# Attention, routed experts and a feed-forward layer in one Trainium2 kernel: values loaded in thirds on one queue, routing in groups of three, single scatters between key copies, and a new order of the last tile

## What is computed

```python
k_sum = k.reshape(B, H, nb, block, D).max(axis=3)
v_sum = v.reshape(B, H, nb, block, D).mean(axis=3)
...
a = a / (np.sum(a, axis=-1, keepdims=True) + 1e-09)
out = np.matmul(a, v_all)
...
logits = x @ w_gate
noise_scale = np.log1p(np.exp(x @ w_noise))
noisy_logits = logits + noise_scale * noise
top2 = np.argpartition(-noisy_logits, 2, axis=1)[:, :2]
...
h = np.maximum(x[mask] @ w1[e], 0.0)
out[mask] += top2_w[mask, k, None] * (h @ w2[e])
...
g = s * (r * r) + b
return g @ w_out
```

## Time and profile before

| | us |
|---|---|
| median of 3 runs (703.12 to 707.35) | 706.74 |
| the profiled execution, its own time | 703.65 |
| its span on the core | 702.0 |
| PE busy in the span | 683.7 (97%) |
| PE's first product of the first expert starts | 103.31 |

### The profile page before, as it was taken

The page is one execution under the profiler, slowest core; times in us unless marked ns, Lnnn a source line. Parts: engine busy times, 40 slices in busy tenths (PEclk is TensorE's granted clock), DMA queues, the critical chain, the costliest instruction groups (busy, mean ns, idle before and its releaser), DMA issues.

```text
span 702.0 us, 10455 instructions
## 1 busy us (share of the span) xinstructions
PE 683.7 (97%) x4065; PEld 569.8 (81%) x4065; DVE 261.0 (37%) x551; ACT 216.1 (31%) x499; POOL 309.4 (44%) x278
## 2 busy tenths in 40 slices
PE   8898989999999999999999999999999999999998
PEld 3466789788888888888999899888888888888886
DVE  6467766431230212312121244944505235051330
ACT  2458955221220311203131313411324113141231
POOL 1415745567988396697889562302021020200000
PEclk9999968999999999999999999999999999999999
DMA  9996433699979195792979599932012020100001
GB/s 261 255 289 183 168 136 134 221 397 362 405 258 400 54 388 197 254 382 76 384 249 397 183 336 315 379 113 61 1 60 61 1 60 1 45 15 1 0 1 60
DMA packets 55966, 132.34 MB, mean 189 GB/s; under 512 B 8712, under 2 KB 11016, under 8 KB 55920
## 3 DMA queue, kind: packets, MB, share of 16 engines
q0 software_dynamic: 28144, 82.77, 33.7%
q1 hardware_dynamic: 27155, 47.77, 20.9%
q10 hardware_dynamic: 621, 1.18, 0.7%
HBM read 104.79 MB, written 25.97 MB: 186 GB/s over the span
## 4 chain that ended last, share of the span: by engine, by line
PE 91%; issue 2%; DMA 2%; ACT 2%; DVE 1%; POOL 1%; SPq 0%; POOLq 0%
PE ps L380 27%; PE ps L382 27%; PE ps L381 27%; PE ps L1531 2%; PE ps L1464 1%; PE ps L1419 1%; DMA v_all<-v_all 1%; PE ps L1447 1%; PE ps L1391 1%; ACT prob L693 1%; PE ps L1427 1%; PE ps L1669 1%; PE ps L1456 1%; POOL kwin L567 1%; POOL x_sorted L582 1%
## 5 line engine op out<-in xcount | busy, mean ns | idle before, releaser
L546 POOL TENSOR_TENSOR w_lo<-w_raw,w_hi 128x1024 fp32r<-128x1024 f32 x56 | 134.2, 2416 | 20.5 <-DMA w_hi<-in_w_pieces_dram 19.7
L967 DVE SCALAR_TENSOR_TENSOR h_lo<-ps,h_hi 128x448 fp32r<-128x448 f32 (+2 forms) x64 | 36.7, 574 | 197.2 <-ACT h_hi L704 197.2
L380 PE MATMUL ps<-x_hi,w_hi 128*128 128x448 f32 (+2 forms) x256 | 88.2, 345 | 0.0
L704 ACT ACTIVATE h_hi<-ps 128x448 fp32r<-128x448 f32 (+2 forms) x64 | 32.3, 505 | 181.0 <-PE ps L382 181.0
L381 PE MATMUL ps<-x_lo,w_hi 128*128 128x448 f32 (+2 forms) x256 | 88.0, 344 | 0.0
L382 PE MATMUL ps<-x_hi,w_lo 128*128 128x448 f32 (+2 forms) x256 | 88.0, 344 | 0.0
L380 PE MATMUL ps<-w_hi,h_hi 128*128 128x512 f32 x216 | 86.8, 402 | 0.0
L382 PE MATMUL ps<-w_hi,h_lo 128*128 128x512 f32 x216 | 84.5, 391 | 0.0
L381 PE MATMUL ps<-w_lo,h_hi 128*128 128x512 f32 x216 | 84.5, 391 | 0.0
L1313 DVE SCALAR_TENSOR_TENSOR sqr<-relu,sbb 128x512 f32<-128x512 f32 x48 | 36.2, 754 | 112.9 <-ACT relu L838 112.2
L381 PE MATMUL ps<-y_lo,w_hi 128*128 128x512 f32 (+1 forms) x200 | 76.1, 381 | 0.0
(11 more groups left out here) (228 smaller groups left out, 1125.0 us busy)
## 6 DMA issues: line engine op xcount, KB each, us to landing
w_raw<-in_w_pieces_dram POOLq DMA_DIRECT2D x56, 512.0 KB, 13.8
w_hi<-in_w_pieces_dram POOLq DMA_DIRECT2D x56, 512.0 KB, 15.3
xb<-x_sorted SPq DMA_DIRECT2D x25, 256.0 KB, 7.5
y_sorted<-ysb SPq DMA_DIRECT2D x25, 256.0 KB, 2.0
x_sorted<-zrow SPq DMA_DIRECT2D x7, 896.0 KB, 15.0
w_raw<-in_w_pieces_dram SPq DMA_DIRECT2D x8, 512.0 KB, 4.7
w_hi<-in_w_in_dram POOLq DMA_DIRECT2D x8, 512.0 KB, 7.8
w_raw<-in_w_in_dram SPq DMA_DIRECT2D x8, 512.0 KB, 8.3
```

Of the source, the lines that this page charges most:

```text
L380: pe.matmul(acc, l_hi, r_hi, start=start, stop=False, skip_group_check=True)
L546: pool.tensor_tensor(piece(w_lo, slot, k), piece(w_raw, slot, k), piece(w_hi, slot, k).bitcast(F32), ALU.subtract).then_inc(pieces_split, 1)
L704: act.activation(hi[:, i // FT % 2, i % FT, 0:rows], ps[:, i % FT, 0:rows], ACT.Relu).then_inc(sg.hhi_ready, 1)
L967: dve.scalar_tensor_tensor(out=lo[:, at, i % FT, 0:rows], in0=ps[:, i % FT, 0:rows], scalar=0.0, in1=hi[:, at, i % FT, 0:rows].bitcast(F32 ...
```

## The change

The mask is loaded ahead of the keys. ACT issues no transfers any more: all values of the first batch are loaded by SP, in three pieces of 4, 4 and 4 windows (the last made of three transfers), each with a semaphore of its own. The rest of the queries waits on SP until the second piece has landed, and the keys of the second batch now come before its values. PE takes each third of the means as it lands. POOL copies four rows of means itself, in two copies, and one of the spreading DMAs is gone. PE's order for tiles 0 to 2 is new, the 50 warming products become 39. Routing goes in four groups of three tiles, `EARLY_TILES` is 6. The first 12 scatters are issued one by one between POOL's key copies, each behind a wait on PE's progress. In the last tile PE turns the probabilities, then x of tile 10, then does the values, ranks and logits; DVE normalises before it reads. Behind it ACT's last logarithm stands ahead of its first `up_early`, DVE's second `up_early` ahead of `split_first(2)`, and the last ranks stand inside `down_early(0)`.

The core of the diff:

```diff
@@ -73,11 +73,10 @@
 HPT = HPB // KD
-GROUP_OF = ((0, 4), (4, 7), (7, 10), (10, 12))
-RANK_BANK = (7, 7, 2, 7)
+GROUP_OF = ((0, 3), (3, 6), (6, 9), (9, 12))
 RAW_AT = (6, 6, 6, 6, 7, 8)
-ROUND_AT = (8, 9, 11)
-GMAX = 4
+ROUND_AT = (8, 10, 11)
+GMAX = 3
@@ -385,16 +384,19 @@
             sp.dma_start(cst[:, :], consts[:, P:]).then_inc(c_in, 16)
+            sp.dma_start(msk[0:80, :], masks[0:80, 0:4 * P]).then_inc(m_in, 16)
             load_keys(sp, 0)
-            sp.dma_start(msk[0:80, :], masks[0:80, 0:4 * P]).then_inc(m_in, 16)
...
             sp.dma_start(ident[:, :], consts[:, 0:P]).then_inc(id_in, 16)
-            load_windows(sp, 0, 0, HPB // 2, v_in[0])
+            for i in range(HPT):
+                load_windows(sp, 0, i * KD, min((i + 1) * KD, HPB - 1), v_third[i])
+            load_last_window(sp, 0, v_third[HPT - 1])
+            sp.dma_start(wg[:, :, :], w_gate.rearrange("(k p) e -> p k e", p=P)).then_inc(g_in, 16)
+            sp.wait_ge(v_third[HPT - 2], 16)
             load_queries(sp, 0, 1)
-            sp.dma_start(wg[:, :, :], w_gate.rearrange("(k p) e -> p k e", p=P)).then_inc(g_in, 16)
-            load_windows(sp, 1, 0, HPB - 1, v_in[1])
-            load_last_window(sp, 1, v_in[1])
             load_keys(sp, 1)
+            load_windows(sp, 1, 0, HPB - 1, v_in)
+            load_last_window(sp, 1, v_in)
@@ -568,19 +570,22 @@
             def spread_means(b):
-                pool.wait_ge(rows_ready, b + 1)
+                pool.wait_ge(rows_ready, 1 if b == 0 else 3)
...
                     pool.wait_ge(pool_win_ready, 4)
-                    pool.tensor_copy(v_all[0][SUMS:COLS, 2:4, :], v_all[0][SUMS:COLS, 0:2, :]).then_inc(rows_copied, 1)
-                for part, (fro, to) in enumerate(((MEANS_BY_DVE[b], 6), (6, HPB))):
+                    for at in (2, 4):
+                        pool.tensor_copy(v_all[0][SUMS:COLS, at:at + 2, :],
+                                         v_all[0][SUMS:COLS, 0, :].unsqueeze(1).broadcast_to([NSUM, 2, DM])).then_inc(rows_copied, 1)
+                for part, (fro, to) in enumerate(((1, 6), (6, HPB))):
+                    if b == 0 and part == 0:
+                        continue
...
-            def scatter(t):
-                for c in range(2):
-                    pool.indirect_dma_start(out=x_sorted, out_offset=bass.IndirectOffsetOnAxis(pos_i[:, t, c:c + 1], 0),
-                                            in_=x_sb[:, t, :], in_offset=None).then_inc(scattered, 16)
+            def scatter(t, c):
+                pool.indirect_dma_start(out=x_sorted, out_offset=bass.IndirectOffsetOnAxis(pos_i[:, t, c:c + 1], 0),
+                                        in_=x_sb[:, t, :], in_offset=None).then_inc(scattered, 16)
@@ -590,21 +595,41 @@
             key_windows(8)
-            key_windows(9)
-            key_windows(10)
...
             pool.wait_ge(pos_ready, 1)
-            for t in range(*GROUP_OF[0]):
-                if t == 2:
-                    key_windows(11)
-                scatter(t)
-            for g in range(1, len(GROUP_OF)):
+            scatter(0, 0)
+            pool.wait_ge(pv_done, 7)
+            scatter(0, 1)
+            key_windows(9)
+            pool.wait_ge(turned, 16)
+            scatter(1, 0)
+            pool.wait_ge(pv_done, 8)
+            scatter(1, 1)
+            key_windows(10)
+            pool.wait_ge(turned, 18)
+            scatter(2, 0)
+            pool.wait_ge(pv_done, 9)
+            scatter(2, 1)
+            pool.wait_ge(pos_ready, 2)
+            scatter(3, 0)
+            key_windows(11)
+            scatter(3, 1)
+            pool.wait_ge(pv_done, 10)
+            scatter(4, 0)
+            pool.wait_ge(scores_done, 12)
+            scatter(4, 1)
+            pool.wait_ge(turned, 22)
+            scatter(5, 0)
+            pool.wait_ge(pv_done, 11)
+            scatter(5, 1)
+            for g in range(2, len(GROUP_OF)):
...
                 for t in range(*GROUP_OF[g]):
-                    scatter(t)
+                    for c in range(2):
+                        scatter(t, c)
@@ -730,9 +755,6 @@
             act.activation(gate[:, :], zrow[:, 0:NT], ACT.Copy)
-            act.wait_ge(k_in[0][PAIRS - 2], 16)
-            load_windows(act, 0, HPB // 2, HPB - 1, v_rest_in)
-            load_last_window(act, 0, v_rest_in)
@@ -740,11 +762,14 @@
                     exps(2)
-                if s >= 1:
+                    act.wait_ge(pv_done, 1)
+                if s >= 3:
...
                                ACT.Copy).then_inc(probT_odd, 1)
+                if s in (1, 2):
+                    x_to_logits(s)
@@ -770,8 +795,8 @@
                 noise_exp(last)
+                noise_ln(last)
                 up_early(0)
-                noise_ln(last)
@@ -1061,50 +1086,50 @@
             mean_weights()
+            masks_to_bf16()
...
             key_sums(1)
-            masks_to_bf16()
...
                     maxima(1)
-                elif s == 1:
-                    maxima(3)
...
                 dve.tensor_copy(probT[0:COLS, 0:4, :], ps[0:COLS, 4, :].rearrange("p (h n) -> p h n", n=P)).then_inc(probT_even, 1)
+                if s == 1:
+                    maxima(3)
                 if s == 0:
+                    copy_means(0)
                     maxima(2)
-                    copy_means(0)
-                    mean_rows(0, 0, 2)
+                    mean_rows(0, 0)
+                    mean_rows(0, 1)
...
                 if s == 4:
-                    mean_rows(1, 0, 1)
+                    mean_rows(1, 0)
                 if s == NT - 1:
-                    route_top(2)
-                    route_chosen(2)
+                    normalise(s)
...
                     read_logits(s - 1)
+                if s in (3, 6, 9):
+                    route_a(s // 3 - 1)
                 if s in (4, 7, 10):
-                    route_a(s // 3 - 1)
-                if s in (5, 8):
                     route_top(s // 3 - 1)
-                if s == 6:
-                    route_c(0)
-                if s == 9:
-                    route_c(1)
+                if s in (5, 8, 11):
+                    route_c(s // 3 - 1)
+                if s == 8:
                     early_count()
-                normalise(s)
-                if s in (5, 8):
+                if s < NT - 1:
+                    normalise(s)
+                if s in (4, 7, 10):
@@ -1117,13 +1142,12 @@
                 x_split(head, i, xa_lo, xa_hi, i, P, 4 + i)
-            route_c(2)
...
             up_early(0)
+            up_early(1)
             split_first(2)
-            up_early(1)
@@ -1475,50 +1500,62 @@
                 for t in range(at, to):
-                    acc = ps[:, RANK_BANK[g], L_RANK + (t - at) * E:L_RANK + (t - at + 1) * E]
+                    acc = ps[:, 7, L_RANK + (t - at) * E:L_RANK + (t - at + 1) * E]
...
-            warm_up(34, 7)
+            warm_up(26, 7)
...
             scores(1)
-            warm_up(8, 7)
+            warm_up(4, 7)
+            mean_third(0, 0)
+            warm_up(6, 7)
...
             scores(2)
-            warm_up(4, 7)
-            means(0)
-            warm_up(4, 7)
+            mean_third(0, 1)
+            mean_third(0, 2)
+            warm_up(3, 7)
             gather_means(0)
+            turn_probs(1)
+            values(0)
             scores(3)
-            values(0)
-            for s in range(1, NT):
-                if 3 < s + 1 < NT:
-                    scores(s + 1)
-                if s == 7:
+            turn_x(0)
+            values(1)
+            logits(0)
+            turn_probs(2)
+            turn_x(1)
+            values(2)
+            logits(1)
+            for s in range(3, NT - 1):
+                scores(s + 1)
+                if s == 6:
                     pe.wait_ge(rank_read, 1)
-                if s == 10:
+                if s == 9:
                     pe.wait_ge(half_ready, 1)
-                if s > 1:
-                    turn_x(s - 1)
+                turn_x(s - 1)
                 turn_probs(s)
-                if s == 1:
-                    turn_x(0)
                 if s == 3:
-                    means(1)
+                    for r in range(HPT):
+                        mean_third(1, r)
...
                     gather_means(1)
-                if s == 6:
+                if s == 5:
...
                     ranks(0)
-                if s == 9:
+                if s == 8:
...
                 values(s)
+            turn_probs(NT - 1)
+            turn_x(NT - 2)
+            values(NT - 1)
+            pe.wait_ge(xT_ready, NT - 1)
             ranks(2)
+            logits(NT - 2)
@@ -1602,13 +1640,15 @@
+                def rank_last(t):
+                    if t == 1:
+                        pe.wait_ge(lg_ready, NT)
+                        ranks(3)
+                        pe.matmul(ps[:, 6, 0:E], ones[:, :], before[:, NT, :], start=True, stop=True).then_inc(counts_done, 1)
...
                 up_early(1)
```

(9 more changed lines are left out.)

61 lines of the change are left out of this document (30 added, 31 removed).

## The result

| | kernel before | changed kernel |
|---|---|---|
| median, us | 706.97 (6 runs, 703.12 to 708.40) | 715.38 (6 runs, 708.99 to 716.93) |
| ratio | | 1.0127, 95% interval 1.0094 to 1.0159 |
| profiled execution, us | 703.65 | 716.93 |
| its span, us | 702.0 | 715.2 |
| mean granted clock | 0.985 | 0.971 |

The time is 1.9 us above the upper end of the range. The profiled executions lie at opposite ends: 703.65 us is close to the fastest of the six runs before, 716.93 is the slowest of the six after.

What follows compares the result with a forecast made beforehand. PE was taken as the bound, without idle time that counts from 130 us on, so earlier losses move the end. Terms -1.0 + 0 + 0.9 + 3.5 + 1.4 = +4.8 on 703.65 gave 708.4 us, range 700 to 713.5.

Steps and rivals of the forecast that it cites:

- A: Opening, to the end of the second batch's means: gain of 1.0 us, bounds a gain of 3.5 and a loss of 0.5.
- rival 3: Slower: the clock falls in PE's wait for the second batch's values, other losses near their upper bounds; 715.0 us, chance 12%.
- threshold: PE waits of 1.35 and 1.42 us left the clock up, 1.59 came before a fall; 2.5 was forecast in the opening.
- B: Tiles 3 to 10, from the second means to the end of tile 10's values: no change, bounds -1.5 to +1.5 us.
- C: Last tile, from tile 10's values to the first expert: loss of 0.9 us, bounds a gain of 5.7 and a loss of 1.7.
- D: Rows of the last group, six scatters for four, ahead of the first expert's second part: loss of 3.5 us, bounds 1.1 and 4.0.
- E: Clock behind PE's wait for the last group's rows: loss of 1.4 us, half of a possible 2.8, bounds 0 and 2.8.
- The walk that gave 43.9: Second means to end of tile 10's values, new order summed tile by tile at today's durations: 43.9 us against 44.4.

Runs made afterwards that it cites:

- a1: The changed kernel, unchanged, run on another chip: 713.75 us against 704.93 for the kernel before, ratio 1.0058, of the medians 1.0125.
- f3: Kernel before with single scatters and the new opening repaired (second batch's values before keys, no SP wait, later key summary): 701.93 us against 704.93, ratio 0.9952.
- f1: Changed kernel with second batch's values before keys, no SP wait, later key summary: 709.50 us against 714.77 (0.9855); on another chip 708.96 against 705.03 (1.0031).
- e3: Changed kernel with 10 products of zeros in PE's wait ahead of the second means: 713.24 us against 705.12 for the kernel before, ratio 1.0100.
- e2: Changed kernel without SP's wait for the second third of the values: 709.43 us against 705.12 for the kernel before, ratio 1.0082.
- h1: Kernel before with the changed kernel's opening; old groups, scatters and last tile: 717.04 us against 714.77, ratio 1.0039.
- b1: The kernel before, unchanged, traced on another chip: 706.34 us in one run, against a median of 704.93 there.
- e1: Changed kernel with the second batch's values issued on SP ahead of its keys: 711.33 us against 705.12 for the kernel before, ratio 1.0127.
- f2: Opening of h1 repaired (values before keys, no SP wait, later key summary), scatters in bursts: 707.88 us against 714.77 (0.9922); again 710.65 against 716.49 (0.9911).
- h3: Kernel before with only the groups of three, single scatters and new last tile: 715.23 us against 714.77 (1.0001); on another chip 713.25 against 705.03 (1.0115).
- f4: f3 with products of zeros in PE's five waits from the end of tile 10's values on: 701.23 us against 716.49 for the kernel before, ratio 0.9788.
- e6: Changed kernel with 14 products of zeros in PE's wait for the last group's rows: 712.16 us against 705.03 for the kernel before, ratio 1.0092.

## Why the prediction was wrong

**The base.** The sum was made against the profiled execution, 703.65, and its result given as the time, while the median of the kernel before was 3.1 higher. Set on the median the same +4.8 is 711.5, inside the range. The spans of the profiled pair differ by 13.2, the medians by 8.4 (8.8 in a1): 3.3 of the miss of 7.0 us is the base, the rest the steps below.

**A, the step that failed.** The step was "PE waits from 39.3 to 41.8, then needs 2.8": a gain of 1.0, measured as a loss of 3.0. In the changed kernel's own trace PE was ready at 43.95 - 3.12 = 40.83, waited until 43.95, and needed 4.68. So 1.5 of the 4.0 us is PE's later readiness (39.10 in f3 and 39.34 in f1), 0.6 a longer wait, and 1.9 the means at the lower clock, which the sum left out. With the loads repaired (f1, f3) the wait and the fall are gone: the means start at 39.34 and 39.10 and take 2.78 us; with zeros in the wait (e3) the fall alone is gone.

The wait was no accident of one trace. In six traces with the change's loads, among them e2's, the second batch's values landed at 40.7, 41.4, 42.0, 43.9, 44.0 and 45.4 us, PE waited 2.8 to 6.2, and each time the clock fell: the means took 3.87 to 5.35 us for 2.78. (In h1 the wait was 1.33 us and the means took 2.78.) I took one landing for a fixed time and left the fall to rival 3 with 12%, on a threshold laid between 1.4 and 1.6 us of idle time on one side and my 2.5 on the other. By that threshold itself the fall should have been in the forecast. The threshold doesn't hold either. Timeline of PE in b1, the kernel before on another chip, at the place of today's fall:

```profile
95.51 0.66 PE L1456 MATMUL ps<-ident,x_sb 128*128 128x128 f32 x4 [1.59 <-DVE x_sb L1002]
```

The wait is the same 1.59 us, but these products took 0.66 us for 0.94, and the clock was 1.00 from 93.92 to 98.10 us; it fell behind a second wait of 1.08. Rival 3 gave 715.0, near the median by luck of the base: its steps sum to 11.3 (A 1.8, B 1.5, C 1.7, D 3.5, E 2.8), the profiled pair to 13.2.

**B.** Of its 3.2 us, 2.9 are the logits, values, masks and scores that follow the means, at the lower clock (6.74 us for 3.87), so they belong to A's fall. But the groups of three aren't free: from the end of the second means to the end of tile 10's values f1 takes 46.3 us, f3, with the old groups, 44.2 and the kernel before 44.4, all three at a mean clock of 0.96. The walk that gave 43.9 was about 2 short. The two parts sum to more than the 3.2 of the pair: there PE was idle for 4.1 us of this stretch against 3.9 before, in f1 for 5.5 against 3.7 in f3. Slower products seem to have filled part of the idle time that the groups make, which no run separates.

**C** held in size: 14.2 us forecast and measured. The values of tile 11 start 5.2 us behind tile 10's end (forecast 5.0), and PE's three gaps are 1.13, 0.72 and 1.22 us (about 1.3). The mean clock was 0.61, where the forecast had all of it at the lower level. Nine more traces with the change's last tile give 11.4 to 14.7, the 11.4 (e1) with the clock at 0.85 in it.

**D** held: 3.5 forecast, 3.6 measured. DVE's `rank_all` came 0.5 us later, counted from the first expert's start (forecast 0.95), and the two added scatters cost 3.0 us (forecast 2.6). It is 2.3 in other pairs (a1's 25.1 against f3's 22.8), where the clock was up earlier. Where no products of zeros were put in this wait, PE idles 4.1 to 4.2 us in every trace with six scatters, 1.1 to 1.8 with four.

**E.** I took half of 2.8 for a fall that might not come. It came in every trace with a wait of 4.1 us or more there. From the turned rows to the end these take 1.2 to 2.5 us more than the kernel before.

**The single scatters** were priced only by their issue time. On a chip of the slow kind DVE stood still over bursts in every trace of a kernel that has them (h1, f2 twice), and the tail that costs 1.15% elsewhere costs nothing there (h3). Single scatters lessen the waits but don't remove them: f1 and h3 have one each on such a chip, f4 three. That the bursts are why the kernel before is slower there is likely, not shown: it was not traced on such a chip. The profile that the prediction rests on has no such wait.

The Trainium skill says in "TensorE: Matmul & The Clock Gate", Part 1, that this clock follows how busy PE has recently been. The traces agree: 0.54 behind the wait of 3.12 us, and 1.00 at the same place in e3, where zeros filled it.

## What to carry to other kernels

Work won ahead of a load is only won if the load is in time: when PE comes earlier, look at what lands when over several traces, and at who else waits in order for the load that is moved back (here DVE's key summaries). A wait on PE longer than those that left the clock up should be priced with the slower products behind it, and can be filled with products of zeros: that kept the clock up behind the wait in e3, e6 and f4, though in e3 half of the gain was lost again at a later fall. Set a sum of differences on the median, not on the one profiled execution.

## What the runs showed of the hardware

- The landing of the same 2.3 MB varied by 4.7 us between traces (40.7 to 45.4). Issuing their large piece 5.1 us earlier (e2) did not bring it out of that range.
- The kernel before took 705 us on three chips and 715 to 716 on two; on the latter DVE and ACT stood up to 7.6 and 7.4 us while GpSimd issued four or six indirect transfers without a pause (h1, f2), but not over the last six in h1. f4, with single scatters there, has three waits of 1.2 to 2.8 us of DVE.
- The clock also fell with idle times near 1 us in front (0.66 between 60 and 70 us in e3, idle 0.92 and 0.42), and stayed up through 1.17 us in the same trace, 1.33 in h1 and 1.59 in b1.
